# MLP token pairs of 504 (four) and 496 (two) tokens a tile in place of 512 (five) and 448

## The reference

```python
scores = (1.0 / S) * np.matmul(z, z.transpose(0, 2, 1))      # z: 2 x 3008 x 64
attn = np.maximum(scores, 0.0) ** 2
x = (u * np.matmul(attn, v)).reshape(B * S, D)               # u, v: 2 x 3008 x 256
h = x @ moe_w_in                                             # 256 x 2048
x = (h - np.tanh(h)) @ moe_w_out                             # 2048 x 256
gate = 1.0 / (1.0 + np.exp(-(x @ moe2_w_gate)))              # 256 x 1536
return gate * (x @ moe2_w_val) @ moe2_w_out                  # 1536 x 256
```

## Time and profile before

| | us |
|---|---|
| median of three runs | 1497.74 (1497.09 to 1497.86) |
| span of the profiled execution, first to last instruction | 1496.5 |
| TensorE busy | 1491.7 |
| TensorE weight loads busy | 1257.0 |
| VectorE busy | 1135.7 |
| ScalarE busy | 949.3 |

### The profile page before, as it was taken

The page is one execution under the profiler, slowest core; times in us unless marked ns, Lnnn a source line. Parts: engine busy times, 40 slices in busy tenths (PEclk is TensorE's granted clock), DMA queues, the critical chain, the costliest instruction groups (busy, mean ns, idle before and its releaser), DMA issues.

```text
span 1496.5 us, 21893 instructions
## 1 busy us (share of the span) xinstructions
PE 1491.7 (100%) x8796; PEld 1257.0 (84%) x8796; DVE 1135.7 (76%) x1417; ACT 949.3 (63%) x1284; POOL 0.5 (0%) x5
## 2 busy tenths in 40 slices
PE   9999999999999999999999999999999999999999
PEld 8888888888888888888888889888888888888898
DVE  8999989999987787777686777666666676666656
ACT  8677767777766666666666666655556555555654
POOL 0000000000000000000000000000000000000000
PEclk9999999999999999999999999999999999999999
DMA  4344422254434345453535446453636454544352
GB/s 141 138 162 154 151 80 89 89 210 159 159 121 171 116 153 187 155 196 131 211 140 184 155 171 236 176 190 127 246 127 217 156 200 172 191 179 190 134 211 88
DMA packets 36341, 241.79 MB, mean 162 GB/s; under 512 B 3600, under 2 KB 6672, under 8 KB 22928
## 3 DMA queue, kind: packets, MB, share of 16 engines
q1 hardware_dynamic: 36096, 240.17, 43.8%
q10 hardware_dynamic: 144, 0.23, 0.0%
HBM read 196.21 MB, written 44.17 MB: 161 GB/s over the span
## 4 chain that ended last, share of the span: by engine, by line
PE 100%; ACT 0%; issue 0%; DVE 0%
PE acc L551 25%; PE hidden L618 13%; PE hidden L623 13%; PE hidden L620 13%; PE acc L511 10%; PE acc L513 10%; PE acc L512 10%; PE hidden L538 6%; PE acc L717 0%; PE acc L731 0%; PE acc L724 0%; ACT part_hi L923 0%; ACT h L920 0%; ACT x_out L1021 0%; DVE part_lo L1149 0%
## 5 line engine op out<-in xcount | busy, mean ns | idle before, releaser
L1030 DVE TENSOR_TENSOR part_lo<-h,part_hi 128x1024 fp32r<-128x1024 f32 (+3 forms) x317 | 375.1, 1183 | 81.8 <-ACT part_hi L870 50.0
L862 ACT ACTIVATE snap<-hidden 128x512 f32<-128x512 f32 (+1 forms) x360 | 211.8, 588 | 250.5 <-PE hidden L623 250.1
L618 PE MATMUL hidden<-region 128*128 128x512 f32 (+1 forms) x840 | 324.0, 386 | 0.0
L620 PE MATMUL hidden<-region 128*128 128x512 f32 (+1 forms) x840 | 323.7, 385 | 0.0
L623 PE MATMUL hidden<-region 128*128 128x512 f32 (+1 forms) x840 | 323.5, 385 | 0.0
L551 PE MATMUL acc<-part_hi,region 64*128 64x512 f32 (+1 forms) x2256 | 286.2, 383 | 0.4 <-ACT part_hi L923 0.4
L1120 DVE TENSOR_TENSOR h<-hidden,snap 128x512 f32<-128x512 f32 (+1 forms) x252 | 170.6, 677 | 143.8 <-ACT snap L862 117.8
L511 PE MATMUL acc<-part_hi,region 128*128 128x512 f32 (+1 forms) x664 | 256.2, 386 | 0.0
L512 PE MATMUL acc<-part_lo,region 128*128 128x512 f32 (+1 forms) x664 | 256.1, 386 | 0.0
L513 PE MATMUL acc<-part_hi,region 128*128 128x512 f32 (+1 forms) x664 | 256.0, 386 | 0.0
L551 PEld LDWEIGHTS acc<-part_hi,region 64*128 64x128 f32 x2256 | 216.5, 184 | 38.6 <-issue 0.8
(11 more groups left out here) (69 smaller groups left out, 1150.5 us busy)
## 6 DMA issues: line engine op xcount, KB each, us to landing
region<-ready SPq DMA_DIRECT2D x33, 2304.0 KB, 8.7
region<-ready SPq DMA_DIRECT2D x51, 1408.0 KB, 5.9
ready<-region SPq DMA_DIRECT2D x6, 2304.0 KB, 7.4
ready<-region SPq DMA_DIRECT2D x8, 1408.0 KB, 5.8
xs<-x_out SPq DMA_DIRECT2D x20, 512.0 KB, 6.1
x_in<-xs SPq DMA_DIRECT2D x20, 512.0 KB, 7.8
snap<-vP SPq DMA_DIRECT2D x24, 256.0 KB, 2.6
u_in<-uT SPq DMA_DIRECT2D x10, 512.0 KB, 5.3
```

The costliest lines, as they stand in the source:

```text
L618: pe.matmul(dst, weights[0], x[0], start=i < 3, stop=False, skip_group_check=True)
L620: pe.matmul(dst, weights[0], x[1], start=False, stop=False, skip_group_check=True)
L862: act.activation(snap[:, g % 2, i, 0:w], hidden[:, CHAIN[g % 2], 0:w], ACT.Copy).then_inc(s_snap, 1)
L1030: return ve.tensor_tensor(dst, whole, hi.bitcast(F32), ALU.subtract)
```

## The change

The widths of the six pairs come from a table instead of from a formula. The sum of the widths, the number of pairs, units and instructions, and every buffer's size and place stay as they were; a tile still begins at a multiple of 512 columns in its buffers in SBUF and PSUM.

```diff
+PAIR_WIDTHS = (504, 504, 504, 504, 496, 496)
+assert len(PAIR_WIDTHS) == PAIRS and 2 * sum(PAIR_WIDTHS) == ALL and max(PAIR_WIDTHS) <= TOK
+
+
 def pair_width(q):
-
-    return min(TOK, (ALL - q % PAIRS * 2 * TOK) // 2)
+    return PAIR_WIDTHS[q % PAIRS]
 
 
 def pair_token(q):
-    return q % PAIRS * 2 * TOK
+    return 2 * sum(PAIR_WIDTHS[:q % PAIRS])
```

## The result

| | before | after |
|---|---|---|
| median of five runs, us | 1497.74 (1497.09 to 1497.86) | 1507.60 (1506.99 to 1508.25) |
| span of the profiled execution, us | 1496.5 | 1505.4 |
| TensorE busy, us | 1491.7 | 1500.0 |

The ratio is 1.0066, with a 95% interval from 1.0056 to 1.0077: slower by 9.9 us, where 3.3 us less had been forecast. The range did not hold the time. The profiled run took 1507.19 us as a whole, 1.8 more than its span, and the same 1.8 stands between the two in every whole kernel of the experiments. So the 1.2 us given for the kernel before, a median less the span of one execution, is not that part: by my estimate its profiled execution took some 1498.3 us.

The account below looks back on a forecast made before the run. TensorE's distance between matmul starts was taken to bound the kernel; −2.4 and −1.0 for the MLPs, with −0.1, +0.1, −0.1 and +0.15, gave −3.35 us, so 1494.4 from 1497.74. The range was 1493.0 to 1497.9 us.

Parts of the forecast that it names:

- token load: Loads for pairs 4 and 5 stay hidden with some 12 us of room, costed at nothing.
- ScalarE's cover in the first pair: In two units of the first pair, late snapshots could lengthen a weight load's wait: +0.1 us, ends 0 and +0.3.
- the last unit: The 0.3 us wait for a low part in the last unit shrinks: −0.1 us.
- The law that I take: Distance between TensorE matmul starts is the larger of columns/2.4 + 13.3 ns and a weight load with handover, 203 to 207 ns.
- the −2.4 us of the first MLP: First MLP's matmuls go from 482.4 to 480.0 us, with 504 at 223.3 and 496 at 220.0 ns.
- the −1.0 of the second: Second MLP's matmuls go from 529.0 to 528.0 us, with 504 at 223.3 and 496 at 220.0 ns.
- The 13.3 ns: Time left over the columns' 213.3 ns in the 226.7 ns distance at 512, taken as fixed above the crossing.
- The short distances of 200 ns inside: First three starts of a second-MLP 448 stretch, 0.20 us apart, read as columns plus the fixed part.
- The floor from the load: In the 448 pairs a 128-column weight load of 188 ns with its handover holds the distance at 203 to 207 ns.
- The third, the special 512: Rival: every width but 512 carries the 20 and 16 ns seen at 448; slower by 17, near 1515 us; chance 0.03.
- The second, steps of 16 columns: Rival: columns are taken in steps of 16, so 504 costs as much as 512 and 496 costs 220; 1504.5 us; chance 0.09.
- the two smooth shapes: The forecast with a proportional-extra rival, 1493.0 to 1495.3 us, chance 0.66; a straight line (1497.7) or late bend, 0.20.

Follow-up runs that it names:

- The stream: Bare streams of 96 float32 matmuls of a kind with weight loads, attention and MLPs left out; 544 cycles at 512 and 504, 536 at 496, 486.4 at 448.
- the sweep: The bare stream run over 23 widths from 512 down to 384, moving operand at offset 0; 508 took 546.2 cycles, 512 took 544, 500 took 536.
- cut_504: Kernel before, but every 512-column matmul of the two MLPs computes only its first 504 columns; 1496.18 us, ratio 0.9991.
- shift_8: Kernel before, with the moving operands of the 448 pairs starting 8 columns later in their buffers; 1498.80 us, ratio 1.0010.
- pairs_500: Changed kernel with pairs of 500 five times, moving operands starting 4 columns later, and 508 once without shift; 1490.03 us, ratio 0.9954 to the kernel before.
- shift_16: Kernel before, with the moving operands of the 448 pairs starting 16 columns later in their buffers; 1494.69 us, ratio 0.9980.
- pairs_480: Changed kernel with pairs of 512 four times and 480 twice; 1499.27 us, ratio 1.0012 to the kernel before.

## Why the prediction was wrong

**What held.** TensorE's distance between starts was the only thing that counted. No token load came late: issued until 639.15 and landing 8.0 us later, against a first reader at 659.27. Nor did ScalarE's cover in the first pair get worse, where I had taken +0.1. The −0.1 for the last unit did not come either: its wait is 0.3 us in both kernels. The two late snapshots, which answer to the earlier trace rows, left a smaller gap:

```profile
537.46 0.19 PEld L621 LDWEIGHTS hidden<-region 128*128 128x128 f32 x1 [0.27 <-ACT snap L865]
...
547.78 0.19 PEld L621 LDWEIGHTS hidden<-region 128*128 128x128 f32 x1 [0.27 <-ACT snap L865]
```

From the last matmul start to the span's end it was 3.6 us before and 3.8 after, within the ends given for that.

**The step that failed** is "The law that I take": columns/2.4 + 13.3 ns or the weight load, whichever is longer. It put 504 at 223.3 ns and 496 at 220.0. They ran at 226.7, and at 223.3 in three of four pairs. In the terms of the sum, the −2.4 us of the first MLP became 360·(4·226.67 + 2·223.3) − 482.4 = +4.8, and the −1.0 of the second became 396·(4·226.67 + 220.0 + 223.3) − 529.0 = +5.6. Both halves of the law were wrong.
- The 13.3 ns were read off one width, 512, where the law was, in the prediction's own words, exact by construction. The stream shows that 512 is one of the few widths at 32 cycles over its columns, and that 36 to 45 is usual at offset 0. The short distances of 200 ns inside I read as a law shining through; they are one part of a repeating pattern with a mean of 202.67.
- The floor from the load was an inference from the earlier trace rows and the small gap between two loads. At 384 columns the stream runs at 174 ns with loads of 188 ns, and loads of 134 and 108 ns don't shorten it at 512. The duration in a load's row bounds nothing by itself.

So the excess of the 448 pairs, 6.65 and 2.6 ns, was not the price of being narrow, and making them wider gave nothing back: 448 sat at 38 to 48 cycles over its columns, 504 sits at 40 and 496 at 32 to 40. The change traded ten pairs at 32 and two at 38 to 48 for eight at 40 and four at 32 to 40. That is the whole sign of the result.

**The rivals.** The third, the special 512, had the right idea, with 0.03; its sizes came from carrying the 448 excess over unchanged, 1515 instead of 1507.6. The second, steps of 16 columns, gave the nearest time, 1504.5, and 504 as the trace shows it, for a reason that the sweep refutes. For two points on a curve I gave 0.86 to the two smooth shapes.

**What stays open** is the mechanism. Shown: bfloat16 has none of it, it needs no other engine, the width and the starts of both operands move it, a shorter load doesn't remove it, and some widths have two steady distances, between which a stream can change behind a stop, behind other matmuls, and in cut_504 in mid-stream. Whether the reads of the two operands get in each other's way, which the places suggest, no run measured. All streams wrote to PSUM in one pattern, so a part of the output in it isn't excluded, though the kernels, with another order of banks, ran at the streams' cycles. What holds a stream of 448 from offset 0 at 496 cycles in one MLP and 486.4 in the other, and why it changed in the cut kernel, isn't settled either.

## What to carry to other kernels

Before the width of a float32 matmul is changed, measure the distance between starts at just that width and place, in a bare stream of a hundred, more than once, since 488, 496 and 500 have more than one steady distance: two widths of a trace say nothing about a third, and the stream foretold shift_8, pairs_500 and shift_16 within 0.1, 0.4 and 0.7 us (as differences to the kernel before on the same chip within 0.1, 0.6 and 0.8), and fits pairs_480, reckoned afterwards, within 0.1. When TensorE's stream is dense, the start of the moving operand in its buffer is a knob worth trying: it brought 2.6 us in shift_16 and cost 1.7 in shift_8. Balancing tile widths was worth nothing in itself here; what counts is the sum of the distances, each at its own width.

## What the runs showed of the hardware that was not expected

- Float32 matmuls with a weight load each of 128 columns have no straight price in the width: 508 columns cost 546.2 cycles, 512 cost 544, 504 cost 544, 500 cost 528 to 549 by offset and history.
- Means like 486.4, 524.8, 501.3 and 533.3 are patterns of five and three matmuls that repeat and whose sum is a multiple of 16 cycles (2432, 2624, 1504, 1600).
- Bfloat16 in the same stream: 6 cycles over the columns from 256 to 512, at 512 from five offsets, with loads of 98 ns where the float32 load takes 188.
- A moving operand of 512 that starts 8 columns off costs 16 cycles, 6.7 ns, more than one at offsets 0, 64, 128, 256 and 384. At 448 columns a multiple of 64 is no safe place: 496 cycles from 64, 486.4 from 0.
- A stream can change from one steady distance to another without a wait: 448 columns went from 486.4 to 496 cycles inside one pair of cut_504.
